# First loads and warm-up matmuls of a convolution and two-MLP kernel: half a window for tile 0, a counting instruction moved, narrower zero matmuls

## The reference, cut to what matters

```
x    = causal 7-tap filter of x (2 x 4096 tokens, 192 channels)   # softmax of the 8 heads' taps
h    = x @ w_in1;  g = h * clip(h + 3, 0, 6) / 6;  x = g @ w_out1   # 192 -> 2048 -> 192
h    = x @ w_in2;  g = where(h > 0, h, exp(min(h, 0)) - 1)
out  = g @ w_out2
```

## Time and profile before

| | |
|---|---|
| Time, median of 3 runs | 1120.34 us (1120.33 to 1121.3) |
| The profiled execution: its own time | 1120.58 us |
| Its span, first to last instruction | 1118.7 us |
| TensorE matmul busy | 1113.0 us (99%) |
| VectorE busy | 901.3 us (81%) |
| ScalarE busy | 633.6 us (57%) |
| GpSimd busy | 39.2 us (4%) |
| DMA, mean over the span | 20 GB/s |

### The profile page before, as it was taken

How to read it: one execution, slowest core, us unless ns; L and a number is a source line. 1 busy time by engine, 2 the same in 40 slices (tenths; PEclk the granted TensorE clock), 3 DMA queues, 4 the chain that set the end, 5 groups by cost and what they waited for, 6 DMA issues and landing times.

```text
span 1118.7 us, 24069 instructions
## 1 busy us (share of the span) xinstructions
PE 1113.0 (99%) x9736; PEld 1014.5 (91%) x9736; DVE 901.3 (81%) x964; ACT 633.6 (57%) x685; POOL 39.2 (4%) x36
## 2 busy tenths in 40 slices
PE   9999999999999999999999999999999999999998
PEld 7999999999999999999999999999999999999997
DVE  8897887878888788787878878788787887876776
ACT  7765646556555554655555555465555655546544
POOL 3422000000000000000000000000000000000000
PEclk9999999999999999999999999999999999999999
DMA  4310010100101001010010100001000010000000
GB/s 158 117 59 10 1 34 0 33 0 0 33 0 33 0 0 33 0 33 0 0 33 0 33 0 1 32 0 33 0 24 9 0 33 0 9 5 11 6 2 29
DMA packets 10664, 22.48 MB, mean 20 GB/s; under 512 B 1424, under 2 KB 1424, under 8 KB 10640
## 3 DMA queue, kind: packets, MB, share of 16 engines
q1 hardware_dynamic: 10496, 22.12, 6.1%
q10 hardware_dynamic: 144, 0.01, 0.0%
HBM read 15.83 MB, written 6.29 MB: 20 GB/s over the span
## 4 chain that ended last, share of the span: by engine, by line
PE 98%; DVE 1%; DMA 0%; issue 0%; ACT 0%; DVEq 0%
PE h_ps L695 31%; PE acc_a L709 31%; PE acc_b L717 21%; PE h_ps L702 15%; DVE conv_a L466 0%; DMA taps<-tap_w 0%; PE h_ps L725 0%; DVE hidden L528 0%; PE acc_a L783 0%; PE acc_a L757 0%; PE acc_b L765 0%; PE acc_b L759 0%; PE acc_b L777 0%; PE acc_a L764 0%; PE acc_a L758 0%
## 5 line engine op out<-in xcount | busy, mean ns | idle before, releaser
L353 ACT CAST g_hi<-hidden 128x1024 fp32r<-128x1024 f32 x255 | 268.8, 1054 | 351.7 <-DVE hidden L533 238.2
L537 DVE TENSOR_TENSOR g_lo<-hidden,g_hi 128x1024 fp32r<-128x1024 f32 x255 | 312.9, 1227 | 127.7 <-ACT g_hi L353 127.7
L695 PE MATMUL h_ps<-in_hi_a,win_hi_a 64*128 64x512 f32 x1012 | 390.7, 386 | 0.0
L709 PE MATMUL acc_a<-g_hi,wout_hi_a 64*128 64x512 f32 x1012 | 390.7, 386 | 0.0
L695 PE MATMUL h_ps<-in_hi_a,win_lo_a 64*128 64x512 f32 x1012 | 390.6, 386 | 0.0
L709 PE MATMUL acc_a<-g_hi,wout_lo_a 64*128 64x512 f32 x1012 | 390.6, 386 | 0.0
L695 PE MATMUL h_ps<-in_lo_a,win_hi_a 64*128 64x512 f32 x1012 | 390.6, 386 | 0.0
L717 PE MATMUL acc_b<-g_hi,wout_b 64*128 64x512 f32 x1012 | 350.3, 386 | 0.0
L709 PE MATMUL acc_a<-g_lo,wout_hi_a 64*128 64x512 f32 x1012 | 310.1, 386 | 0.0
L717 PE MATMUL acc_b<-g_lo,wout_b 64*128 64x512 f32 x1012 | 310.0, 386 | 0.0
L528 DVE SCALAR_TENSOR_TENSOR hidden<-hidden,h_ps 128x1024 f32<-128x1024 f32 x128 | 156.3, 1221 | 59.0 <-ACT hidden L343 58.8
(11 more groups left out here) (112 smaller groups left out, 1212.9 us busy)
## 6 DMA issues: line engine op xcount, KB each, us to landing
xwin_a<-x_win SPq DMA_DIRECT2D x16, 259.0 KB, 2.8
raw_in<-w_in SPq DMA_DIRECT2D x8, 512.0 KB, 3.6
out_t<-out_a SPq DMA_DIRECT2D x16, 256.0 KB, 2.9
xwin_b<-x_win SPq DMA_DIRECT2D x15, 259.0 KB, 2.9
raw_out<-w_out SPq DMA_DIRECT2D x8, 384.0 KB, 3.9
out_t<-out_b SPq DMA_DIRECT2D x16, 128.0 KB, 2.3
xnext_b<-x_win SPq DMA_DIRECT2D x1, 259.0 KB, 5.5
taps<-tap_w ACTq DMA_DIRECT2D x1, 7.0 KB, 2.6
```

The lines of the kernel that those rows point to most:

```text
L353: nc.scalar.copy(g_hi[:, g % PARTS, :], hidden[:, g % 2, :]).then_inc(hi_ready, 1)
L537: nc.vector.tensor_tensor(g_lo[:, g % PARTS, :], hidden[:, g % 2, :], g_hi[:, g % PARTS, :].bitcast(F32), ALU.subtract).then_inc(lo_ready, 1)
L695: return nc.tensor.matmul(bank(g, c), w[HALVES[r], columns(g, c)], x[HALVES[r], :], start=start, stop=c == 0 and r == 1 and term == 2)
L709: return nc.tensor.matmul(acc_a[acc][:, :], w[HALVES[r], g * CPG + c, :], x[HALVES[r], g % PARTS, c * TOK:(c + 1) * TOK], start=g == 0 and ...
```

## The change

Tile 0's part b is loaded from a new input, `x_first`, of 128 rows and 262 columns: rows 0-63 hold the window columns 0 to 261, and rows 64-127 the window columns 256 to 517. So both token halves lie at the same columns of `xwin_b`, and `conv_rest` gets the distance between the halves as an argument (0 for tile 0, 256 for tile 1). The `nop` stands behind the load of weight piece 1. The cleared block is 128 columns wide, and seven matmuls of 128 moving columns take the place of three of 256 and one of 128.

```diff
-            sp.nop().then_inc(stored, 32)
             sp.dma_start(xwin_a[:, :], window(0)[0:DA, :]).then_inc(x0a_loaded, 16)
-            sp.dma_start(xwin_b[:, :], window(0)[DA:DA + 2 * DB, :]).then_inc(x0b_loaded, 16)
+            sp.dma_start(xwin_b[:, 0:HALF + TAPS - 1], x_first[:, :]).then_inc(x0b_loaded, 16)
             load_piece(0)
             sp.dma_start(xnext_b[:, :], window(1)[DA:DA + 2 * DB, :]).then_inc(x1b_loaded, 16)
             load_piece(1)
+            sp.nop().then_inc(stored, 32)
...
-            nc.vector.memset(conv_b[:, 0:HALF], 0.0).then_inc(zero_set, 1)
+            nc.vector.memset(conv_b[:, 0:P], 0.0).then_inc(zero_set, 1)
...
-            def conv_rest(window, banks, taken):
+            def conv_rest(window, second, banks, taken):
...
-                                              window[HALVES[r], r * HALF + k:r * HALF + k + HALF],
+                                              window[HALVES[r], r * second + k:r * second + k + HALF],
...
-                for c in range(2 * CPG):
-                    n = HALF if c < 3 else HALF // 2
-                    nc.tensor.matmul(bank(0, c % 2)[:, 0:n], conv_b[:, 0:P], conv_b[:, 0:n], start=True, stop=True)
+                for c in range(7):
+                    nc.tensor.matmul(bank(0, c % 2)[:, 0:P], conv_b[:, 0:P], conv_b[:, 0:P], start=True, stop=True)
                 pe.wait_ge(x0b_loaded, 16)
-                conv_rest(xwin_b, (bank(1, 0), bank(1, 1)), TAPS)
+                conv_rest(xwin_b, 0, (bank(1, 0), bank(1, 1)), TAPS)
                 pe.wait_ge(x1b_loaded, 16)
-                conv_rest(xnext_b, (acc_a[0], acc_b[0]), PE_TAPS)
+                conv_rest(xnext_b, HALF, (acc_a[0], acc_b[0]), PE_TAPS)
...
+        "x_first": np.ascontiguousarray(np.concatenate([x_win[0, DA:D, 0:HALF + TAPS - 1], x_win[0, DA:D, HALF:WIN]])),
```

More of the change, by code:

```diff
@@ L60, with build @@
 PE_TAPS = 5
-def build(nc, x_win, tap_w, w_in1, w_out1, w_in2, w_out2, out_t):
+def build(nc, x_win, x_first, tap_w, w_in1, w_out1, w_in2, w_out2, out_t):
     w_in, w_out = (w_in1, w_in2), (w_out1, w_out2)
```

## The result

The changed kernel takes 1122.33 us (median of 22 runs, 1120.91 to 1124.61) against 1120.82 us (22 runs, 1120.33 to 1121.51). The ratio is 1.0014, with an interval of 1.0008 to 1.002: slower, by 1.5 us or 0.14%. The forecast was 1120.3 us, no change, with a range up to 1121.9. So the loss lies within the 0.2% that was called "the same", and is real all the same; the time is outside the range and the direction was missed.

The account below looks back on a forecast made before the run. Taken as bound by the taps' DMA and VectorE up to the nonlinearity, then TensorE back to back. TensorE's filter ending 0.04 us sooner gave 1120.34 - 0.04 = 1120.3 us, no change; range 1119.4 to 1121.9.

Parts of the forecast that it names:

- What bounds the kernel: First 15 us: taps' DMA, then VectorE up to the nonlinearity; TensorE back to back after; the change can gain 0.09 us.
- The memset and the zero matmuls: Start of TensorE: zeros start at 1.07 instead of 1.20, passes 0.21 us apart, ending at about 4.17 instead of 4.30.
- Rival C: Zero matmuls: weight loads bound the narrow passes at 0.337 us each, filter about 1.0 us later, median 1121.3; chance 0.06.
- The half load: Tile 0 part b lands at about 4.04 instead of 4.36, first cast at 6.7; TensorE's filter ends only 0.04 us sooner.
- The nop: SyncE's queue: 17 ns, moved behind later loads; worth nothing; bounds zero and part a's whole transfer, 0.64 us; zero taken.
- rival B: Taps' load: part a's packets overtake it, moving the chain one for one, 0.05 to 0.64 us, 1120.4 to 1120.9; chance 0.13.
- The clock: TensorE's rise from 1.2 to 2.4 GHz in the filter: said to vary by half a us from run to run in both kernels.
- Rival D: TensorE's filters: clock rises later or never under narrow matmuls, up to some 4.6 us, 1125; chance 0.05.
- The sum: Whole kernel: filter ends 0.04 us sooner and the chain follows, -0.04 us (ends 0 and -0.09), with 1.9 us around the span.

Follow-up runs that it names:

- e9: The kernel before with two more nops ahead of SyncE's loads, which the compiled program left out, so the kernel before again: 1120.86 us.
- e5: The changed kernel with nine zero matmuls of 128 columns in place of seven: 1120.93 us.
- e13: The changed kernel with the memset and zero matmuls of the kernel before: 1120.80 us.
- e16: The kernel before with its 896 zero columns in eight matmuls of 112 instead of four matmuls: 1121.95 us.
- e1: The kernel before with only the nop moved behind the load of weight piece 1: 1121.02 us.
- e14: The changed kernel with nine zero matmuls of 100 columns in place of seven of 128: 1121.61 us.

## Why the prediction was wrong

*What bounds the kernel* was right: nothing changed behind the nonlinearity, and the loss in the span is the nonlinearity's delay to 0.1 us. That VectorE allows 0.09 us and TensorE's filter is close behind was right for the one execution it was read from; it means that the filter had hardly any slack against a delay, and this side of it wasn't priced. In another execution of the kernel before (e9), where the clock rose 1.3 us later, the filter is already the bound, by 0.81 us:

```profile
9.73 0.75 DVE L569 SCALAR_TENSOR_TENSOR in_lo_b<-h_ps,tap_stat,in_hi_b 128x512 fp32r<-128x512 f32 x1 [0.81 <-ACT in_hi_b L371]
```

*The memset and the zero matmuls:* the passes are 0.21 us apart and cover their loads, as forecast; they start at 1.06 (forecast 1.07) and end at 4.21 (4.17). Rival C was rightly held off.

*The half load* lands at 1.20 + 2.8 = 4.0 us (forecast 4.04) and is worth nothing, as forecast. The first cast of the weights starts at 7.16 us, not at 6.7; it is hidden, as forecast.

*The nop* is the step that failed: "worth nothing ... I take zero". It delayed the taps by 0.56 us in the profiled execution, within the 0.64 that rival B had as its upper price. The evidence was in the trace of before: two issues 0.07 us apart, on one of which the whole chain rests. But B's "moves the chain one for one" doesn't hold on average either. e5 and e13 have the taps 0.5 us late and a mean span of 1119.1, and the kernel before beside them 1119.0 and 1119.15. Only their shortest span moved, to 1118.8 from 1118.5 and 1118.6. A likely reason, not tested, is that in many executions of the kernel before the filter is already the bound, as in e9, and a delay of VectorE hides behind it.

*The clock* was the second failure, and the dearer one. Rivals B and D were taken as separate, each with a small chance. In fact the one can bring on the other: with late taps and the new zeros TensorE stands idle, and in about half of the runs the clock then rises late, in the profiled executions about four us later, 1.87 us of filter. Rival D looked only at the narrow matmuls and said "the pauses no longer than before". The prediction's own numbers speak against it: zeros done at 4.17 and the filter from 4.52 leave 0.35 us, where its numbers of before, 4.30 and 4.58, leave 0.28; with late taps it is 0.96 in the profiled execution. The Trainium skill (TensorE: Matmul & The Clock Gate, section What you observe) lets the rise vary by half a us from run to run. The measurement goes far beyond it: 5.0 to 6.5 us in three executions of the kernel before, 5.0 and 9.6 in two of the changed kernel.

*The sum* had no term for what lies outside the span, taken as 1.9 us in both kernels. It is 0.51 us more on average, a third of the loss, and e16 shows it without the nop, the half load or the narrow memset. In place of the forecast -0.04 us stand +1.06 in the span and +0.51 outside it.

## What to carry to other kernels

Before an instruction is moved in a queue, look at which other engine issues a DMA within 0.1 us of it: the small load that a chain hangs on should be issued first, and a no-op of 17 ns can be what keeps it so. Let warm-up matmuls last until the real ones start: nine of 128 columns left no late span in 22 runs, seven with late taps 17 in 33. Two edits that leave the span alone, each by itself, can meet in one wait, so price them together. Take spans and times apart run by run: a median hides a loss that strikes half of the runs, and time outside the span can change with the mere number of instructions.

## What was not expected of the hardware

- How often the clock rises late goes with what TensorE did in the first 5 us: none of 147 spans of the kernel before is late, with a pause of 0.27 us; 2 of 22 with 0.73 (e1, e13), 17 of 33 with 0.66 to 0.96 after narrower zeros that end 0.14 us earlier, 9 of 11 after only five zero matmuls. A late rise costs 2.2 us of span (1121.2 against 1119.0).
- At 1.2 GHz a float32 pass with its own load of 128 weight columns takes 0.21 us for 100 (e14) and 112 columns (e16, below) as for 128.

```profile
L862 PEld LDWEIGHTS h_ps<-conv_b x16: 288/333/338, 1.2 to 4.4; 128*128 128x128 f32 x16
```

- A load of 7 KB took 2.8 to 3.1 us when a load of 259 KB was issued in the same moment by another engine, and 2.0 to 2.6 when that one came 0.07 us later.
- Three or four more matmuls at the start of TensorE's program put about 0.9 us more behind the last instruction in 44 of 77 runs; one more or five more did not.
